# A chunked recurrence on one core: round 0 of each solve in another PSUM bank behind one copy, v's four transposes together, the state's transposes in the next octet

## The reference, cut to what matters

```python
def _attn_ref(r, k, v, w, a, b):            # all [B=4, H=8, S=768, D=40], fp32
    state = zeros(B, H, D, D)
    for t in range(S):
        y[:, :, t] = einsum('bhd,bhde->bhe', rt, state)
        Sa = einsum('bhde,bhe->bhd', state, at)
        state = state * wt[:, :, None, :] - einsum('bhd,bhe->bhde', Sa, bt)
        state = state + einsum('bhd,bhe->bhde', vt, kt)
...
x = attn_out.transpose(0, 2, 1, 3).reshape(B * S, H * D)      # 3072 x 320
x = _moe_ref(x, ...)       # gate, 8 Sinkhorn rounds, 8 experts 320 -> 1024 -> 320
return _moe2_ref(x, ...)   # 320 -> 2048 (ELU) -> 320
```

## Time and profile before

| what | value |
|---|---|
| median of 3 runs | 2210.52 us (2209.01 to 2212.04) |
| profiled execution | 2208.46 us |
| its span | 2206.5 us |
| recurrence, up to the first product of the feed-forward part | 483.87 us |
| one octet of the middle chunks, start to start | 19.40 us |
| one octet of the first chunk, start to start | 19.03 us |
| TensorE busy, 200 to 250 us | 49.70 of 50 us |
| VectorE / ScalarE / GpSimd busy, 200 to 250 us | 37.35 / 17.69 / 17.92 us |

### The profile page before, as it was taken

The page is one execution under the profiler, slowest core; times in us unless marked ns, Lnnn a source line. Parts: engine busy times, 40 slices in busy tenths (PEclk is TensorE's granted clock), DMA queues, the critical chain, the costliest instruction groups (busy, mean ns, idle before and its releaser), DMA issues.

```text
span 2206.5 us, 35862 instructions
## 1 busy us (share of the span) xinstructions
PE 2174.1 (99%) x14692; PEld 1953.3 (89%) x14692; DVE 1350.8 (61%) x2429; ACT 809.0 (37%) x1429; POOL 408.4 (19%) x376
## 2 busy tenths in 40 slices
PE   7999999989999999999999999999999999999999
PEld 6899999878898998999999999999999998899898
DVE  6777777763466655555555555555555555666665
ACT  3433333333223333333333333333333333433333
POOL 4433333311143111111111111111111010110100
PEclk9999999999999999999999999999999999999999
DMA  6333334321101000000000000000000000000001
GB/s 102 60 63 59 55 64 64 63 81 44 46 20 46 27 1 27 27 1 27 27 1 27 27 1 27 27 1 27 27 1 27 27 1 27 1 27 27 1 14 59
DMA packets 193781, 70.49 MB, mean 32 GB/s; under 512 B 153424, under 2 KB 189776, under 8 KB 193616
## 3 DMA queue, kind: packets, MB, share of 16 engines
q1 hardware_dynamic: 193616, 68.19, 14.0%
HBM read 60.31 MB, written 7.86 MB: 31 GB/s over the span
## 4 chain that ended last, share of the span: by engine, by line
PE 97%; DVE 2%; ACT 0%; issue 0%; POOL 0%; DMA 0%; SPq 0%; DVEq 0%; ACTq 0%; POOLq 0%
PE up L1377 19%; PE up L1336 12%; PE yps L1434 9%; PE yps L1436 9%; PE yps L1435 9%; PE up L1384 7%; PE misc L1153 6%; PE yps L1353 4%; PE yps L1351 4%; PE yps L1352 4%; PE yps L1112 3%; PE up L1127 2%; PE up L1085 2%; PE up L1112 1%; PE yps L1192 1%; PE misc L1146 1%
## 5 line engine op out<-in xcount | busy, mean ns | idle before, releaser
L1884 DVE SCALAR_TENSOR_TENSOR tok<-yps,prob,tok 128x320 f32<-128x320 f32 x672 | 343.2, 547 | 134.7 <-PE yps L1436 134.5
L1434 PE MATMUL yps<-w2h,hh 128*128 128x320 f32 x1344 | 414.9, 309 | 0.3 <-DVE hl L1867 0.3
L1436 PE MATMUL yps<-w2h,hl 128*128 128x320 f32 x1344 | 415.1, 309 | 0.0
L1435 PE MATMUL yps<-w2l,hh 128*128 128x320 f32 x1344 | 415.0, 309 | 0.0
L881 ACT ACTIVATE up<-up 128x512 f32<-128x512 f32 x252 | 146.7, 582 | 396.4 <-PE up L1377 394.8
L1434 PEld LDWEIGHTS yps<-w2h,hh 128*128 128x128 f32 x1344 | 252.5, 188 | 21.7 <-issue 0.8
L1435 PEld LDWEIGHTS yps<-w2l,hh 128*128 128x128 f32 x1344 | 252.3, 188 | 10.6
L1436 PEld LDWEIGHTS yps<-w2h,hl 128*128 128x128 f32 x1344 | 252.3, 188 | 0.0
L686 POOL TENSOR_TENSOR w1l<-w1l_raw,w1h 128x768 fp32r<-128x768 f32 x68 | 103.1, 1516 | 621.2 <-ACT w1h L792 621.2
L1867 DVE SCALAR_TENSOR_TENSOR hl<-up,hh 128x512 fp32r<-128x512 f32 x168 | 115.5, 688 | 161.3 <-ACT hh L893 161.2
L1867 DVE SCALAR_TENSOR_TENSOR hl<-hl_raw,hh 128x512 fp32r<-128x512 f32 x168 | 116.8, 695 | 147.7 <-ACT hh L893 147.7
(11 more groups left out here) (236 smaller groups left out, 4238.5 us busy)
## 6 DMA issues: line engine op xcount, KB each, us to landing
w2l_raw<-in_moe_w SPq DMA_DIRECT2D x16, 640.0 KB, 5.7
w1l_raw<-in_moe_w SPq DMA_DIRECT2D x32, 256.0 KB, 3.0
xr_raw<-x_dram SPq DMA_DIRECT2D x12, 512.0 KB, 4.1
w1l_raw<-in_moe_w SPq DMA_DIRECT2D x32, 128.0 KB, 3.7
wp<-in_w SPq DMA_DIRECT2D x24, 160.0 KB, 3.2
rp<-in_r SPq DMA_DIRECT2D x24, 160.0 KB, 3.1
vp<-in_v SPq DMA_DIRECT2D x48, 80.0 KB, 3.2
raw<-in_a SPq DMA_DIRECT2D x24, 160.0 KB, 3.7
```

The source lines that it names most:

```text
L1434: nc.tensor.matmul(o, hh[:, tile, c], wh, start=first, stop=False)
L1435: nc.tensor.matmul(o, hh[:, tile, c], wl, start=False, stop=False)
L1436: ins = nc.tensor.matmul(o, hl[:, tile, c], wh, start=False, stop=last)
L1884: nc.vector.scalar_tensor_tensor(out=acc, in0=yps[:, s, 0:DM], scalar=prob_of(blk * NSUB + s, e), in1=acc, op0=ALU.mult, op1=ALU.add).then ...
```

## The change

Three edits, all in the order in which TensorE and ACT do the octet's work:

1. Round 0 (`x_b` x `n_b`) is written into bank `pu` and no longer into `pz`, and it waits for one of ACT's two copies of x (`2 * o + 1`) where it waited for both. DVE's first subtraction reads `pu` and still waits for both copies.
2. The transposes of the next octet's v were two before round 1 and two before round 3; now all four stand before round 1.
3. The transposes of the new state (`mt` to `mb`) stood at the end of the octet, ahead of the products of `a_t` and `b_t`; they now stand in the next octet, between the state update's first products and round 3. ACT's copy moves with them, from after k's copy to between v's and r's. The wait for `c_s` (DVE has read the update out of `pu`) stays ahead of `a_t` x `b_t`. The number of such jobs is the same, 20.

The core of the diff (left out: the same renumbering of jobs in POOL's `chunk`, and in the wait behind the last octet):

```diff
-    JOBS = 10
+    JOBS = 9
+    UPDATES = OCT - B
...
+        def jobs_before(o):
+            return T0 + o * JOBS + min(max(o - 1, 0), UPDATES)
...
                     previous(tj, *following)
                     channels(tj, v_t)
+                    if 0 <= g * B + bb - 1 < UPDATES:
+                        job(tj, mb[0:PR, (bb - 1) % B, :, 0:PR], lambda bank: pairs(PR)(bank)[:, :, 0:PR])
                     channels(tj, r_t[:, following[1] % 2])
                     channels(tj, a_t, pw)
...
                     channels(tj, k_t)
-                if not last:
-                    job(tj, mb[0:PR, bb, :, 0:PR], lambda bank: pairs(PR)(bank)[:, :, 0:PR])
...
+            def state_by_rows(tj, o):
+                pe.wait_ge(c_s, o + 1)
+                bank = job_bank(tj)
+                for p in range(PAIRS):
+                    ins = nc.tensor.transpose(bank[0:PR, p * P:p * P + PR], mt[0:PR, o % B, p, 0:PR],
+                                              ident[0:PR, 0:PR])
+                ins.then_inc(c_tj, 1)
...
                 pe.wait_ge(c_nb, 2 * o + 2)
-                pe.wait_ge(c_xc, 2 * o + 2)
-                round_of(n_b, x_b)
+                pe.wait_ge(c_xc, 2 * o + 1)
+                by_head(pu, n_b, x_b, first=True, last=True).then_inc(c_zj, 1)
                 if following:
                     w_by_tokens(tj, *following)
                     pe.wait_ge(c_rv[1 - buf], fills(*following) * 3 * 16)
-                    v_bank = job_bank(tj)
-                    slots_of_pairs(v_bank, vp[:, 1 - buf], range(PAIRS // 2))
+                    slots_by_channels(tj, vp[:, 1 - buf])
...
-                if following:
-                    slots_of_pairs(v_bank, vp[:, 1 - buf], range(PAIRS // 2, PAIRS)).then_inc(c_tj, 1)
+                if 0 <= o - 1 < UPDATES:
+                    state_by_rows(tj, o - 1)
                 pe.wait_ge(c_za, o * ROUNDS + 3)
                 round_of(n_b, z_b)
...
                 if not last:
                     pe.wait_ge(c_s, o + 1)
-                    bank = job_bank(tj)
-                    for p in range(PAIRS):
-                        ins = nc.tensor.transpose(bank[0:PR, p * P:p * P + PR], mt[0:PR, bb, p, 0:PR],
-                                                  ident[0:PR, 0:PR])
-                    ins.then_inc(c_tj, 1)
...
+            zps_first = pu.rearrange("p (i q d) -> p i q d", i=PAIRS, q=2)[:, :, :, 0:D]
...
-                nc.vector.tensor_tensor(filled(z_b), x_pairs, zps, ALU.subtract).then_inc(c_za, 1)
+                nc.vector.tensor_tensor(filled(z_b), x_pairs, zps_first, ALU.subtract).then_inc(c_za, 1)
```

More of the change, by code:

```diff
@@ L688, in chunk @@
             def chunk(g, last=False):
-                jobs = JOBS - 1 if last else JOBS
                 for bb in range(B):
-                    base = g * (B * JOBS) + T0 + bb * jobs
+                    base = jobs_before(g * B + bb)
                     later_only(base - 1, g, bb)
@@ L1265, in _ @@
             chunk(NG - 1, True)
-            pe.wait_ge(c_ta, T0 + (OCT - B) * JOBS + (B - 1) * (JOBS - 1) + 1)
+            pe.wait_ge(c_ta, jobs_before(OCT - 1) + 1)
             pe.wait_ge(c_ya, OCT)
```

## The result

The changed kernel takes 2197.18 us (median of 6 runs, 2194.5 to 2197.61) against 2210.29 us before (median of 6 runs, 2209.01 to 2212.04). The ratio is 0.9939, with a 95% interval from 0.9926 to 0.9952: 13.1 us faster. Forecast were 13.2 us and 2197.3 us. A second set of runs gave 2196.95 us and 0.9942 (0.9929 to 0.9956).

A forecast was written before the change was run, and what follows sets the result against it. TensorE, 97% of the chain, bounds the kernel, with hidden waits. Middle octets 9.3, first chunk 3.0 and last chunk 0.9 sum to 13.2 us, taking 2210.52 to 2197.3; range 2194.5 to 2202.

The forecast's parts named there:

- (a): Middle octet, between `y_state` and round 0: TensorE waits 0.22, with round 0 following ACT's later copy `xf`.
- (b): Middle octet, between two transposes of v and round 1: TensorE waits 0.23, behind DVE's `z_b`.
- (c): Middle octet, between two transposes of v and round 3: TensorE waits 0.17, behind DVE's second `z_b`.
- `y_state` to round 1, 0.22: Middle octets: TensorE's work and DVE's chain, the two arms, meet; round 1 begins 0.22 earlier with two more transposes.
- Round 2 to round 3, at no cost: Middle octets: TensorE's work of 3.14 with the state's transposes fits under DVE's 3.17, 0.03 to spare; cost 0.
- The octet's end, 0.36: Middle octets, before `a_t` x `b_t`: removing the state's transposes saves 0.36 of 0.45; 0.09 stays with the tiling switch.
- First chunk, 3.0: First four octets: 0.33 for octet 0, 0.75 for three octets (w's transposes 0.05 late), 0.47 at the fourth's end.
- Last chunk: Last four octets: no update or state transposes at the ends, so only 0.22 four times, 0.9 us.
- Poor overlap: Rounds 1 and 3: regrouped transposes cost their records' length, 5.8 lost, median 2203.1; chance 0.14 together with DVE's rival.
- DVE at the end: Octet's end: DVE sets it, so 0.36 and 0.47 gain nothing, median 2204.8; chance 0.14 together with poor overlap.
- The job banks: ACT's state copy delays the sa transposes' bank; 1.5 us late per octet would make it slower by 4.4; slower 0.04.
- The clock: After the last octet: a longer stretch at 1.2 GHz moves the time by 1 or 2 us; no separate chance.

The follow-up runs named there:

- Both copies: Changed kernel, but round 0 waits for both of ACT's copies of x again: 2201.49 us, ratio to before 0.9965.
- state behind round 3: Changed kernel with the state's four transposes moved on TensorE from ahead of round 3 to behind it: 2204.13 us, ratio to before 0.9976.
- v split: Changed kernel with v's transposes split again, two before round 1 and two before round 3: 2200.82 us, ratio to before 0.9959.
- edit 1 alone: Kernel before plus only round 0 in the update's bank behind one copy; v split and state's transposes as before: 2203.27 us, ratio 0.9968.
- edit 1 with 2: Changed kernel with the state's transposes and ACT's copy put back at the octet's end: 2202.34 us, ratio to before 0.9963.
- version with two moves: Changed kernel; last chunk only, `rv_t` x `kt` goes behind round 2 and `a_state` ahead of `sa_t`'s products: 2194.29 us, ratio to before 0.993.

## Why the prediction was right

*The bound.* TensorE carries 97% of the chain before and after. Nearly all of the gain came out of waits that its busy share doesn't show; only the 0.33 ahead of round 0 in the first chunk stood in a bracket of its products. In the middle chunks those brackets were empty, but not the brackets of the weight loads of the same three rounds. They stand as PEld in the timeline of all engines before:

```profile
237.80 0.46 PEld L1153 LDWEIGHTS misc<-x_b,n_b 128*128 128x128 bf16 x8 [0.21 <-issue]
...
239.09 0.45 PEld L1153 LDWEIGHTS misc<-z_b,n_b 128*128 128x128 bf16 x8 [0.30 <-DVE z_b L1605]
...
243.82 0.45 PEld L1153 LDWEIGHTS misc<-z_b,n_b 128*128 128x128 bf16 x8 [0.23 <-DVE z_b L1615]
```

The three are the places (a), (b) and (c), two of them with their cause. In the changed kernel these brackets are gone.

*`y_state` to round 1, 0.22.* Measured 0.21. Round 0 follows `y_state`'s end, and both arms meet at round 1, as worked out (2.15 forecast, 2.16 found). "Both copies" takes this back.

*Round 2 to round 3, at no cost.* 3.16 after 3.17. The margin of 0.03 was real: two more transposes made it 3.35 or 3.36.

*The octet's end, 0.36.* Measured 0.35 and 0.54 for k's group, not 0.44: the 0.09 stays with the change from transposes to 40-row products. By the Trainium skill, "TensorEngine Tiling (Array Packing)", Key Properties, that would be the drain at a change of tiling mode; the traces agree with the place, 0.09 or 0.10 each time, but show no cause. The same border shows once more behind it: `a_t` x `b_t` holds TensorE for 0.99 (243.54 to 244.53) and `a_t` x `k_t` for 0.90. Both parts stay where they are, so the sum is not touched.

*DVE's margin at the end.* The prediction has DVE free at the end of the reduction's record, 231.35, with 0.03 to spare. By the 0.39 from start to start that DVE needs where it alone sets the pace, it was free for `n_t` at 231.27, with 0.11 to spare. That fits what was found: TensorE still releases `n_t` (1.19 behind `a_t` x `b_t`). In "state behind round 3" `n_t` stands 0.39 behind the reduction in the middle octets too. An octet is 18.83 (18.8 forecast).

*First chunk, 3.0.* 0.80 an octet (19.03 to 18.23) instead of 0.75: the scan did not come late. The prediction read that DVE had no gap there, by the same record. But `n_t` stood 1.19 behind `a_t` x `b_t` (56.33 to 57.52) and 0.48 behind the reduction (57.04), so TensorE released it and DVE had 0.09 in hand. With that, the 0.05 of lateness becomes 0.04 of margin. "State behind round 3" pushed it over. Against this, the end of the fourth octet gave 0.35 and not 0.47: it already has `a_state` between b's and k's transposes and no wait for b's copy, as a middle octet.

*Last chunk.* 0.21 an octet for 0.22.

*The sum.* Between the rounds 0, 12.87 was forecast and 12.70 measured. The middle octets lack 0.01 each; the two misses of the first chunk, +0.13 and -0.12, cancel by luck.

*The price of a transpose.* The Trainium skill, "TensorE: Matmul & The Clock Gate", Part 4, has 275 ns in a kernel's context. Here v's four hold TensorE for at most 0.46 and the state's four for at most 0.38, and two added ones delayed round 3 by 0.20, not by 0.5. The page's figure fits the length of a record.

*The rivals.* Poor overlap: no, each regrouped batch cost its start-to-start price to 0.02. DVE at the end: no, with more room than was thought. The job banks: not in the changed kernel, but in the version with v split, through v's copy instead of the state's. The clock: the stretches outside the rounds differed by 1 to 2 us between single executions, as allowed for, and made the first pair of profiles show 11.0. Behind the recurrence the granted clock did read 0.50 to 0.88, as before.

*How the three edits share 12.70.* Between the rounds 0, edit 1 alone gives 5.25, edit 1 with 2 gives 5.24, edit 2 with 3 gives 7.54, edit 1 with 3 gives 7.46, all three 12.70. (Round 0 stays in `pu` in the version called edit 2 with 3.) Edit 2 is worth nothing but for clearing the place into which edit 3 moves the state's transposes, and there it is worth 5.24. Edit 3 by itself and edit 2 by itself were not run.

## What to carry to other kernels

When an in-order engine reads as 99% busy, take start-to-start prices from places without a wait, subtract them, and look for distances that are too long; here 0.6 us of each 19.4 us octet lay in them and no idle bracket of a product named it. Look at the weight loads' brackets as well, which did, and read the other engines from start to start too: their margins come out too small by their records. Work may be moved under another engine's chain as long as the sum of those prices stays below the chain, to a few hundredths; here nothing was gained by moving it elsewhere. Before moving a step, follow what the moved step stood between: in the last chunk `a_state` had been covering ACT's copy of b.

## What the runs showed of the hardware that I had not expected

The eight products `r_t` x `sa_t` hold TensorE for 1.09 from start to start whether POOL's b, which the next group needs, is ready 0.8 or 0.4 behind their start (changed kernel and "state behind round 3"), while the eight products `a_t` x `k_t` between two groups of their own kind hold it for 0.90 (431.28 to 432.17 in the version with two moves is 0.89). So a border between 128-row and 40-row products costs some 0.1 in the group behind it, and as much in the group ahead of it: `a_t` x `b_t`, with a border only ahead of it, holds TensorE for 0.99.

A DVE operation ran at about half its speed where POOL had started first. The rows are of "state behind round 3", all engines:

```profile
244.35 0.86 POOL L659 TENSOR_TENSOR kt<-raw,winv 128x320 f32<-128x320 f32 x1
244.61 0.95 DVE L1637 TENSOR_TENSOR mt<-mtmp,wend 104x320 f32<-104x320 f32 x1
```

In that version it is so in octets 1 to 19, 0.95 or 0.96 each time. In the changed kernel DVE's same operation starts first (by 0.12) and takes 0.51, and it is POOL's that takes 1.11 or 1.12; in the last chunk, where there is no such DVE operation, POOL's takes 0.86. Who comes first keeps its speed, in these pairs.
